# One-core attention and two feed-forward layers: three PSUM banks for the first up-product, one for the second, and a division kept in PSUM

## The reference

```
qn, kn = q / (norm(q, axis=1) + 1e-6), k / (norm(k, axis=1) + 1e-6)
s = kn.T @ qn / tau ; A = softmax(s, last axis) ; x = v @ A
h = x @ w_in
P = a0 + a1*h + a2*h^2 + a3*h^3
Q = 1 + |b0|*|h| + |b1|*h^2
y = (P / (Q + 1e-6)) @ w_out
h2 = y @ w_in2
out = (h2 * clip(h2 + 3, 0, 6) / 6) @ w_out2
```

## Time and profile before

| what | value |
|---|---|
| time, median of three runs | 1240.01 us (1239.28 to 1241.65) |
| span of the profiled execution, which stands for its own time | 1240.4 us |
| TensorE busy | 1165.5 us, 94% |
| VectorE busy | 1156.9 us, 93% |
| ScalarE busy | 961.1 us, 77% |
| GpSimd busy | 360.6 us, 29% |
| mean granted TensorE clock | 0.983 of full |
| line 777 on VectorE, 208 times | 206.0 us, mean 991 ns |

### The profile page before, as it was taken

How to read it: one execution, slowest core, us unless ns; L and a number is a source line. 1 busy time by engine, 2 the same in 40 slices (tenths; PEclk the granted TensorE clock), 3 DMA queues, 4 the chain that set the end, 5 groups by cost and what they waited for, 6 DMA issues and landing times.

```text
span 1240.4 us, 17387 instructions
## 1 busy us (share of the span) xinstructions
PE 1165.5 (94%) x5440; PEld 954.5 (77%) x5440; DVE 1156.9 (93%) x1723; ACT 961.1 (77%) x1782; POOL 360.6 (29%) x276
## 2 busy tenths in 40 slices
PE   7876788899999999999999999999999999999998
PEld 6755566787787787787787787787787787888898
DVE  5779999999999999999999999999999999999872
ACT  6566787888887887887887887887887887787864
POOL 2146576222222222222222222222222222222334
PEclk9887899999999999999999999999999999999999
DMA  9730000000000000000000000000000000000000
GB/s 319 265 111 1 18 1 1 1 26 1 1 34 1 0 34 0 0 34 0 0 34 0 0 34 0 0 34 0 0 34 1 1 31 1 1 26 1 18 1 22
DMA packets 16210, 33.65 MB, mean 27 GB/s; under 512 B 1824, under 2 KB 6176, under 8 KB 15904
## 3 DMA queue, kind: packets, MB, share of 16 engines
q1 hardware_dynamic: 16160, 33.04, 7.5%
HBM read 26.87 MB, written 6.16 MB: 27 GB/s over the span
## 4 chain that ended last, share of the span: by engine, by line
PE 41%; DVE 37%; issue 18%; ACT 3%; DMA 0%; DVEq 0%; SPq 0%; POOL 0%; ACTq 0%
DVE T L771 7%; PE H L334 6%; DVE G L784 6%; DVE T L750 6%; PE H L336 6%; PE H L335 6%; DVE SQ L764 5%; DVE R L798 5%; DVE g_lo L792 4%; PE OP L343 3%; PE OP L334 3%; PE OP L336 3%; PE OP L335 3%; PE YP L334 3%; PE YP L336 3%
## 5 line engine op out<-in xcount | busy, mean ns | idle before, releaser
L307 POOL TENSOR_TENSOR g_lo<-R,g_hi 128x512 fp32r<-128x512 f32 (+2 forms) x208 | 267.1, 1285 | 754.9 <-ACT g_hi L598 754.9
L563 ACT ACTIVATE T<-H,coef 128x512 f32<-128x512 f32 (+2 forms) x208 | 153.0, 735 | 161.0 <-PE H L336 160.9
L777 DVE SCALAR_TENSOR_TENSOR Y<-SQ,Y 128x512 f32<-128x512 f32 (+2 forms) x208 | 206.0, 991 | 0.5
L334 PE MATMUL H<-vT_hi,wf_hi 128*128 128x512 f32 (+2 forms) x416 | 159.8, 384 | 20.6 <-DVE T L756 15.2
L334 PE MATMUL H<-yT_hi,wu_hi 128*128 128x512 f32 (+2 forms) x416 | 157.7, 379 | 11.2 <-DVE R L798 10.5
L764 DVE TENSOR_TENSOR SQ<-SQ,AB 128x512 f32<-128x512 f32 (+2 forms) x192 | 167.4, 872 | 0.0
L334 PE MATMUL YP<-g_hi,wd_hi 128*128 128x512 f32 (+2 forms) x416 | 160.0, 385 | 6.3 <-DVE yT_lo L804 5.6
L771 DVE SCALAR_TENSOR_TENSOR T<-T,coef,Y 128x512 f32<-128x512 f32 (+2 forms) x208 | 163.0, 784 | 0.0
L334 PE MATMUL OP<-g_hi,wd_hi 128*128 128x512 f32 (+2 forms) x416 | 156.8, 377 | 1.8 <-ACT o_tok L621 1.5
L336 PE MATMUL YP<-g_hi,wd_lo 128*128 128x512 f32 (+2 forms) x416 | 157.0, 377 | 0.0
L335 PE MATMUL YP<-g_lo,wd_hi 128*128 128x512 f32 (+2 forms) x416 | 156.9, 377 | 0.0
(11 more groups left out here) (89 smaller groups left out, 2259.6 us busy)
## 6 DMA issues: line engine op xcount, KB each, us to landing
qk<-in_q SPq DMA_DIRECT2D x23, 256.0 KB, 5.6
qk<-in_k SPq DMA_DIRECT2D x23, 256.0 KB, 7.0
v_raw<-in_v SPq DMA_DIRECT2D x10, 512.0 KB, 3.6
out<-o_tok SPq DMA_DIRECT2D x10, 512.0 KB, 3.7
w_raw_b<-in_moe_w_out SPq DMA_DIRECT2D x8, 512.0 KB, 5.7
w_raw_a<-in_moe_w_in SPq DMA_DIRECT2D x1, 2048.0 KB, 11.5
w_raw_b<-in_moe_w_in SPq DMA_DIRECT2D x4, 512.0 KB, 6.1
v_raw<-in_v SPq DMA_DIRECT2D x2, 256.0 KB, 7.1
```

Source lines behind the costliest of these rows:

```text
L307: nc.gpsimd.tensor_tensor(g2_lo[:, j % 4, 0:w], R[:, j % 4, 0:w], g2_hi[:, j % 4, 0:w].bitcast(fp32), ALU.subtract).then_inc(g2_lo_done, 1)
L334: nc.tensor.matmul(psum, w_hi, x_hi, start=first, stop=False)
L563: nc.scalar.activation(T[:, j % 4, 0:w], H1[:, j % 2, 0:w], ACT.Identity, bias=A2, scale=A3)
L777: nc.vector.scalar_tensor_tensor(Y[:, j % 2, 0:w], SQ[:, j % 4, 0:w], Q_CONST, Y[:, j % 2, 0:w], ALU.add, ALU.mult).then_inc(e_done, 1)
```

## The change

H1 gets three banks and H2 one (up2 now waits for the gate of one chunk before; only in the last block its odd chunks use H1). A ring of 18 places a step, sixteen chunks and two transposes of the next v, which now follow up1 of slots 4 and 10, turns through H1's banks; a bank is given back when quotient_lo or the v split has read it. v's parts have two buffers.

The division is another: horner_1 writes P - A0 back into the chunk's bank; quotient_hi = (P) * Y is written by VectorE straight as g1_hi; product is Q times it, rest is P less the product (into the bank), quotient_lo is rest * Y, as g1_lo. It runs one slot behind up1, and down1 follows three behind up1, up2 four slots into the next step (six before), down2 two behind up2. T has two buffers, SQ four, AB and Y two, and each waits for its own last reader. GpSimd does q_body in every step, and g2_split in the same slot as the gate, behind a wait for product. down2 has the tokens' part as the stationary operand and is done in 12 products of 256 columns; its sum has tokens on the partitions, so both the transposes of the output and one of the two copies are gone, and the factor 1/6 goes into the copy left. The fold uses OP in place of H2. On SP the load of v is issued a step earlier, behind the store.

The core of the diff (the removed VectorE functions and step bodies are those printed above):

```
-    LAG_ROOT = 1
-    LAG_NEWTON = 2
-    LAG_SPLIT1 = 3
-    LAG_DOWN1 = 5
+    LAG_DIVIDE = 1
+    LAG_DOWN1 = 3
     SHIFT2 = LAG_DOWN1 + 1
-    LAG_DOWN2 = 3
-    POOL_SUMS = 1,
+    LAG_DOWN2 = 2
+    V_BEHIND = 4, 10
...
+    RING = 3
...
-        T = sb("T", [P, 4, W], fp32)
-        G = sb("G", [P, 2, W], fp32)
+        T = sb("T", [P, 2, W], fp32)
         SQ = sb("SQ", [P, 4, W], fp32)
         AB = sb("AB", [P, 2, W], fp32)
...
-        H1, H2, YP, OP = ps("H1"), ps("H2"), ps("YP"), ps("OP")
...
+        H1, H2, YP, OP = ps("H1", RING), ps("H2", 1), ps("YP", 2), ps("OP", 2)
...
+        def place(j):
+            return j + sum(j > a for a in V_BEHIND)
+        def v_place(c):
+            return V_BEHIND[c] + 1 + c
...
+        def bank(at):
+            return at % RING
+        def wait_bank(engine, t, at):
+            before = at - RING
+            t, before = t + before // TURN, before % TURN
+            if not exists(t):
+                return
+            for c in range(CT):
+                if v_place(c) == before:
+                    if exists(t + 1):
+                        engine.wait_ge(vT_lo_done, CT * (t + 1) + c + 1)
+                    return
+            j = before - sum(before > v_place(c) for c in range(CT))
+            wait_chunk(engine, g1_lo_done, (t, j))
+        def h2(blk, j):
+            last = isinstance(blk, int) and blk == NB - 1
+            return (H1 if last and j % 2 else H2)[:, 0, 0:width(blk)]
...
+            def step(t, par):
                 if exists(t - 2):
                     m = width(t - 2) // P
                     sp.wait_ge(o_copied, t - 1)
                     sp.dma_start(tokens_of(out, t - 2, m), o_tok[:, 0:m, :]).then_inc(out_stored, 16)
+                if exists(t + 2):
+                    load_v(t + 2)
...
                 for j in range(J):
+                    if exists(t):
+                        q_body(t, j)
                     if isinstance(t, int) and t == 0:
                         for k in (1, 2):
                             if W_SLOTS[k - 1] <= j < W_SLOTS[k - 1] + 4:
                                 weight_lo(k, j - W_SLOTS[k - 1])
+                    if x := stage(t - 1, j - SHIFT2):
+                        if y := stage(t, j - LAG_DIVIDE):
+                            wait_chunk(pool, product_done, y)
                         g2_split(*x)
...
-                if at := back(blk, j, 2):
+                if at := back(blk, j, 2 if isinstance(blk, int) and blk == NB - 1 and j else 1):
                     wait_chunk(pe, g2_done, at)
...
-                    done = split_product(H2[:, j % 2, 0:w], wu2_hi[:, c, cols], wu2_lo[:, c, cols],
+                    done = split_product(h2(blk, j), wu2_hi[:, c, cols], wu2_lo[:, c, cols],
...
-                for d in range(CT):
-                    done = split_product(OP[:, d, 0:w], wd2_hi[:, j, d * P:(d + 1) * P],
-                                         wd2_lo[:, j, d * P:(d + 1) * P], g2_hi[:, j % 4, 0:w],
-                                         g2_lo[:, j % 4, 0:w], j == 0, j == J - 1)
+                for i in range(w // P):
+                    at = slice(i * P, (i + 1) * P)
+                    psum = OP[:, i // 2, i % 2 * C:(i % 2 + 1) * C]
+                    first, last = j == 0 and i % 2 == 0, j == J - 1
+                    nc.tensor.matmul(psum, g2_hi[:, j % 4, at], wd2_hi[:, j, :], start=first, stop=False,
+                                     skip_group_check=True)
+                    nc.tensor.matmul(psum, g2_hi[:, j % 4, at], wd2_lo[:, j, :], start=False, stop=False,
+                                     skip_group_check=True)
+                    done = nc.tensor.matmul(psum, g2_lo[:, j % 4, at], wd2_hi[:, j, :], start=False, stop=last,
+                                            skip_group_check=True)
...
                 for j in range(J):
...
+                    if x := stage(t - 1, j - SHIFT2):
+                        up2(*x)
                     if exists(t):
+                        up1(t, j, par)
                         if isinstance(t, int) and t == 0 and j in PIECE_AT[:-1]:
                             fold(PIECE_AT.index(j) + 1)
+                        if j in V_BEHIND and exists(t + 1):
+                            if j == V_BEHIND[0]:
+                                pe.wait_ge(v_in, 16 * (t + 2))
+                            transpose_v(t + 1, V_BEHIND.index(j))
+                    if x := stage(t - 1, j - SHIFT2 - LAG_DOWN2):
+                        down2(*x)
+                    if x := stage(t, j - LAG_DOWN1):
+                        down1(*x)
...
             def a1(t, j):
                 w = width(t)
+                h = H1[:, bank(place(j)), 0:w]
                 wait_chunk(act, u1_done, (t, j))
+                wait_chunk(act, t3_done, back(t, j, 2))
+                nc.scalar.activation(T[:, j % 2, 0:w], h, ACT.Identity, bias=A2, scale=A3)
+                wait_chunk(act, rest_done, back(t, j, 4))
+                nc.scalar.activation(SQ[:, j % 4, 0:w], h, ACT.Square, scale=root_b1)
                 wait_chunk(act, w_done, back(t, j, 2))
...
+                nc.scalar.activation(AB[:, j % 2, 0:w], h, ACT.Abs, scale=absb[:, 0:1]).then_inc(a1_done, 1)
             def root(blk, j):
                 w = width(blk)
                 wait_chunk(act, w_done, (blk, j))
+                wait_chunk(act, g1_lo_done, back(blk, j, 2))
                 nc.scalar.activation(Y[:, j % 2, 0:w], SQ[:, j % 4, 0:w], ACT.Abs_reciprocal_sqrt, bias=Q_CONST)\
...
+            def step(t, par):
                 for j in range(J):
...
+                    if j == LAG_DOWN1 and exists(t - 1):
+                        yT_split(t - 1)
                     if u2:
                         c1(*u2)
+                    if exists(t):
+                        a1(t, j)
+                        if j in V_BEHIND and exists(t + 1):
+                            vT_split(t + 1, V_BEHIND.index(j), 1 - par)
+                    if x := stage(t, j - LAG_DIVIDE):
                         root(*x)
                         root_squared(*x)
+                    if u2:
+                        c2(*u2)
+                    if j == OUT_SLOT and exists(t - 2):
                         out_copy(t - 2)
...
             def horner_2(t, j):
                 w = width(t)
                 wait_chunk(dve, a1_done, (t, j))
+                nc.vector.tensor_tensor(T[:, j % 2, 0:w], T[:, j % 2, 0:w], H1[:, bank(place(j)), 0:w], ALU.mult)\
                   .then_inc(t2_done, 1)
             def horner_1(t, j):
                 w = width(t)
+                h = H1[:, bank(place(j)), 0:w]
                 wait_chunk(dve, t2_done, (t, j))
...
+                nc.vector.scalar_tensor_tensor(h, T[:, j % 2, 0:w], A1, h, ALU.add, ALU.mult).then_inc(t3_done, 1)
+            def quotient_hi(blk, j):
                 w = width(blk)
                 wait_chunk(dve, y2_done, (blk, j))
                 wait_chunk(dve, t3_done, (blk, j))
...
+                wait_chunk(dve, d1_done, back(blk, j, 4))
+                nc.vector.scalar_tensor_tensor(g1_hi[:, j % 4, 0:w], H1[:, bank(place(j)), 0:w], A0, Y[:, j % 2, 0:w],
+                                               ALU.add, ALU.mult).then_inc(g1_hi_done, 1)
+            def product(blk, j):
                 w = width(blk)
                 wait_chunk(dve, g1_hi_done, (blk, j))
...
+                nc.vector.scalar_tensor_tensor(SQ[:, j % 4, 0:w], SQ[:, j % 4, 0:w], Q_CONST,
+                                               g1_hi[:, j % 4, 0:w].bitcast(fp32),
+                                               ALU.add, ALU.mult).then_inc(product_done, 1)
+            def rest(blk, j):
+                w = width(blk)
+                p = H1[:, bank(place(j)), 0:w]
+                wait_chunk(dve, product_done, (blk, j))
+                nc.vector.scalar_tensor_tensor(p, p, A0, SQ[:, j % 4, 0:w], ALU.add, ALU.subtract)\
+                  .then_inc(rest_done, 1)
+            def quotient_lo(blk, j):
+                w = width(blk)
+                wait_chunk(dve, rest_done, (blk, j))
+                nc.vector.tensor_tensor(g1_lo[:, j % 4, 0:w], H1[:, bank(place(j)), 0:w], Y[:, j % 2, 0:w], ALU.mult)\
+                  .then_inc(g1_lo_done, 1)
             def gate2(blk, j):
                 w = width(blk)
                 wait_chunk(dve, r_done, (blk, j))
+                nc.vector.scalar_tensor_tensor(R[:, j % 4, 0:w], R[:, j % 4, 0:w], 6.0, h2(blk, j),
...
+                    if j == LAG_DOWN1 and exists(t - 1):
+                        yT_split(t - 1)
+                    if exists(t):
+                        horner_2(t, j)
+                        horner_1(t, j)
+                        if j in V_BEHIND and exists(t + 1):
+                            vT_split(t + 1, V_BEHIND.index(j), 1 - par)
+                    if x := stage(t, j - LAG_DIVIDE):
+                        quotient_hi(*x)
+                        product(*x)
+                        rest(*x)
```

(68 more changed lines are left out.)

193 lines of the change are left out of this document (33 added, 160 removed).

## The result

The changed kernel takes 2185.58 us (median of four runs, 2182.44 to 2187.34) where the kernel before took 1240.83 on the same chip: a ratio of 1.76, with a 95% interval of 1.757 to 1.763. The forecast was 2170, slower.

The account below looks back on a forecast made before the run. TensorE's 24 products (5.6 us a slot) bound the kernel, VectorE needing about as much. A 9.33 us circle plus 1.7 for the clock gives 11.0 a slot; 66 + 60 + 135 + 173 + 1419 + 152 + 118 + 46 = 2169, say 2170 us (1860 to 2320).

Parts of the forecast that it names:

- The circle: Each slot: up2 waits for the gate, which stands behind a1 and VectorE's queue; 9.33 us a slot at full clock.
- Unpriced operations: VectorE's PSUM writes priced like reads, some -30 to +45 us; product beside GpSimd charged nothing, 120 us more if they meet.
- The clock: TensorE's 3.5 us pauses lower its clock in every slot, costing 1.7 us (ends 0 and 2.4): 11.0 us a slot.
- full-clock rival: TensorE's clock stays full despite the 3.5 us pauses: 1868 us, chance 0.11.
- always-low one: TensorE's clock is low throughout, slots of 11.7 us: 2299 us, chance 0.10.
- The sum, term by term: Whole kernel, from the start through block 0 and the steps to the end: 2169, say 2170 us.
- block 0: Its 16 slots of 256 tokens have no gate circle: 60 us, for 64.7 before the change.
- the rest: Behind step 11: step 12 at 118 us and the end at 46, one transposition and one copy fewer.
- The other parts of a full step: Split of y in slot 3 adds 0.2 us, splits of v in slots 4 and 10 0.6 each: 1.4 a step.
- The signs: up2 waits some 3 us over 150 times, T starts 9.3 to 11.7 us apart, middle clock 0.7 to 0.85.
- Edits at nothing: Parts charged nothing, among them earlier releases of T, AB, SQ and Y, and down products fitting in TensorE's pause.
- The faster rival: The circle doesn't close since the gate is ready before up2; TensorE's 24 products bound the slot: 1205 us, chance 0.02.

Follow-up runs that it names:

- filler12: Changed kernel with twelve products whose result is overwritten added on TensorE ahead of up2 in 12 of 16 slots: 1977.47 us.
- gate_mid: Changed kernel with VectorE's gate moved up by three operations, behind horner_1 and before quotient_hi: 1585.63 us.
- quotient_first: Changed kernel with VectorE's gate, then the four quotient operations, ahead of horner_2 and horner_1, and ScalarE's root and root_squared ahead of a1: 1208.12 us.
- lag4: Changed kernel with down1 four slots behind up1 instead of three and up2 five slots into the next step instead of four: 2180.6 us.

## Why the prediction was right

- **The circle.** Right in place and size. Horner_2 to the gate's end was summed as 4.25 less 0.05; measured 4.24. a1 with the way to VectorE 1.98; measured 1.97. The slot at full clock 9.33; filler12 has 9.37. gate_mid's slot was 7.18 by the same terms and is 7.20.
- **Unpriced operations.** Writing PSUM costs nothing that can be seen: horner_1 and rest last 0.76, the reading of the earlier trace rows was 0.75. Product lasts 0.69 in the blocks of 512 tokens and in the changed kernel never met GpSimd from step 1 on, as argued. In block 0 it did, six times, for 1.4 to 2.0 us in place of 0.42: the prediction counted GpSimd's sums and subtractions of activations and left out the weights' remainders, which wait for no product.
- **The clock.** 1.7 us a slot forecast. Measured 1.5 in the usual slot and 2.4 in the slots of the long low stretches; over steps 3 to 10 it is (179.1 - 16 x 9.37 - 1.3 for the splits) / 16 = 1.7. That the mean came out so exactly is partly luck, since no row had shown a low stretch of 6.8 us in steady work. With 127 falls in the 128 slots of steps 3 to 10 the throttling is paid about once a slot, and the full-clock rival (1868 us) and the always-low one (2299) both fall. The Trainium skill (TensorE: Matmul & The Clock Gate, section "HAM oscillation — how this bites in real kernels") describes a kernel whose bursts of products are parted by long waits and which pays for it at every burst. The trace agrees, with a fall at 1158.2 and the next at 1168.5.
- **The sum, term by term** (forecast, measured): start 66, 64.7; block 0 60, 77.0; step 1 135, 137.4; step 2 173, 176.8; steps 3 to 10 1419, 1433.1; step 11 152, 140.5; the rest 164, 152.9. That the total is within 1% owes something to errors of both signs. The largest error for its size is block 0: I let it gain 5 us, since it has no gate circle, and it lost 12. What it has instead is the ring of three banks, for which the forecast has no term: TensorE's first products into H1, up1's and the transposes', wait for quotient_lo, 20.9 us in all:

```profile
PE H L357 <- DVE g_lo L776: 15.9, 9, 4.5
...
PE H L397 <- DVE g_lo L776: 5.0, 2, 4.6
```

The block further depends on when T, SQ and AB are released (88.7 without the early releases), on the order of the queues (67.7 in quotient_first) and on the product beside GpSimd; how the 12 us are divided among these stays open. Steps 11 and 12 I had with the clock term of the others; five of step 11's 16 slots take 8.0 us, the full-clock sum, and the mean clock of either step is 0.89.

- **The other parts of a full step**: forecast 1.4 us, and the step is 179.1 - 16 x 10.9 = 4.7 above 16 usual slots. Five or six slots of 16 take 11.4 to 12.4 us. The splits have 0.6 us each in it, as forecast (12.38 beside 11.79); the other 3.5 are the clock's, in slots whose low stretch covers all twelve products.
- **The signs.** 190 waits of 3.2 us at up2, a granted clock of 0.80 from 460 to 1885 us, VectorE waiting for Abs for half of the time and GpSimd busy for 24% came as said. T starts 10.7 to 12.4 us apart in steps 3 to 10, which is above the 11.7 named as the end, since a split and a long low stretch can fall into one slot.
- **Edits at nothing.** The lag: lag4, no change. The releases: nothing in the circle, 17 us outside it. The faster rival (circle open, 1205 us) was wrong for this kernel and right for the same operations in another order: 1208.

## What to carry to other kernels

When a buffer is cut from two to one, the producer's wait reaches into the same slot. Then follow every engine's queue, not only that of the waiting one: whatever stands between the consumer and the operations that need the producer's next neighbour closes a circle, and its length is the new slot. Here it could close at three places in two queues, TensorE's and ScalarE's, and reordering at one only moved it to the next. Moving the consumer ahead of the rest of its slot took most of it away (1374 us), and the quotient ahead of horner as well, on both engines, the rest (1208 us). And if an engine with a throttled clock gets a pause in each slot, price its clock as well: here it was 1.5 of the 5.3 us that the usual slot lost.

## What the runs showed of the hardware

- Useless products can pay: 12 more in a slot of 24 gave 208 us of 2186 back, by keeping TensorE's clock at 2.4 GHz.
- With pauses of 3.1 to 3.7 us in every slot of some 11 the clock fell 127 times in 128 slots (changed kernel, steps 3 to 10), for 3.4 us or for 6.8; with pauses of 1.3 us in slots of 7.2 (gate_mid) it did not fall from 460 to 1582 us.
- The turn of a loop of two steps cost TensorE two pauses of 1.2 us in the mean (quotient_first), which the unrolled kernel does not have.
- A VectorE operation that reads SBUF twice took 1.4 to 2.0 us beside GpSimd's subtraction of 1024 columns, and 0.42 alone (L760 at 256 columns, block 0 of the changed kernel).
